# The k'v product of the batch two on follows the mean squares; four pairs of banks; the rest tokens go ahead of the fourth row tile

## The reference, cut to what matters

```
kv  = einsum('bhsd,bhse->bhde', k, v)              # 8 heads of 64; no softmax
out = einsum('bhsd,bhde->bhse', q, kv)
x   = out / sqrt(mean(out*out, -1) + 1e-6) * g_norm       # then heads side by side: [8, 576, 512]
u, v = split(relu(x @ w_in), 2, axis=-1)                  # 512 columns each
v_n  = (v - mean(v)) / sqrt(var(v) + 1e-6)
v_s  = einsum('ts,bsd->btd', w_spatial, v_n) + b_spatial[:, None]
y    = (u * v_s) @ w_out
h    = relu(y @ w_in2)                                    # w_out @ w_in2 is formed once
conv = three taps over the tokens of h
result = (h * sigmoid(conv)) @ w_out2
```

## Time and profile before

| | |
|---|---|
| median of 3 runs | 794.38 us (793.95 to 794.77) |
| the profiled execution's own time | 794.56 us |
| its span in the trace | 792.5 us |
| PE busy / ACT busy / DVE busy | 781.0 / 421.9 / 584.9 us |
| granted TensorE clock | full speed |
| one body of the steady loop | 47.0 us |

### The profile page before, as it was taken

How to read it: one execution, slowest core, us unless ns; L and a number is a source line. 1 busy time by engine, 2 the same in 40 slices (tenths; PEclk the granted TensorE clock), 3 DMA queues, 4 the chain that set the end, 5 groups by cost and what they waited for, 6 DMA issues and landing times.

```text
span 792.5 us, 15400 instructions
## 1 busy us (share of the span) xinstructions
PE 781.0 (99%) x5654; PEld 702.0 (89%) x5654; DVE 584.9 (74%) x1262; ACT 421.9 (53%) x753; POOL 29.5 (4%) x40
## 2 busy tenths in 40 slices
PE   8999999999999999999999999999999999999997
PEld 7679889798988979899899898898989999898986
DVE  3666776776577475666889989497995979679791
ACT  3664462544335254352556767366674756557562
POOL 4342000000000000000000000000000000000000
PEclk9999999999999999999999999999999999999999
DMA  9872455856334272222091213222022212102101
GB/s 316 308 256 61 150 199 193 301 181 224 105 103 181 74 268 60 104 51 80 36 355 67 105 54 105 67 75 84 1 105 67 104 53 86 71 13 105 53 0 66
DMA packets 35001, 96.86 MB, mean 122 GB/s; under 512 B 2738, under 2 KB 9106, under 8 KB 30228
## 3 DMA queue, kind: packets, MB, share of 16 engines
q1 hardware_dynamic: 33476, 90.09, 33.2%
q10 hardware_dynamic: 1488, 6.30, 2.1%
HBM read 66.11 MB, written 30.28 MB: 122 GB/s over the span
## 4 chain that ended last, share of the span: by engine, by line
PE 89%; DVE 6%; DMA 1%; ACT 1%; issue 1%; SPq 0%; DVEq 0%; ACTq 0%
PE ps L619 25%; PE ps L443 24%; PE ps L611 21%; PE ps L474 11%; PE ps L396 3%; PE ps L412 2%; PE ps L544 1%; DMA kv_raw<-kv_rest_dram 1%; PE ps L422 1%; DVE t_then_s L1148 1%; DVE bn_stats L1067 1%; DVE work L1087 1%; DVE v_hg_split L1093 1%; DVE vrr L1080 0%; PE ps L532 0%
## 5 line engine op out<-in xcount | busy, mean ns | idle before, releaser
L619 PE MATMUL ps<-w_in_split,v_hg_split 128*128 128x512 f32 x832 | 194.9, 390 | 0.0
L619 PEld LDWEIGHTS ps<-w_in_split,v_hg_split 128*128 128x128 f32 x832 | 155.7, 188 | 32.2
L443 PE MATMUL ps<-w_sp_split,v_hg_split 128*128 128x288 f32 x896 | 120.5, 295 | 1.0 <-DVE v_hg_split L1095 0.6
L443 PEld LDWEIGHTS ps<-w_sp_split,v_hg_split 128*128 128x128 f32 x896 | 119.3, 188 | 1.5 <-issue 0.8
L443 PE MATMUL ps<-x_operand_split,w_in_split 128*128 128x288 f32 x768 | 104.3, 296 | 1.6 <-ACT work L701 1.6
L443 PEld LDWEIGHTS ps<-x_operand_split,w_in_split 128*128 128x128 f32 x768 | 102.1, 188 | 3.7 <-ACT work L701 2.0
L474 PE MATMUL ps<-w_in_split,x_operand_split 128*128 128x512 f32 x384 | 93.6, 397 | 0.0
L474 PEld LDWEIGHTS ps<-w_in_split,x_operand_split 128*128 128x128 f32 x384 | 70.4, 188 | 20.9 <-issue 6.1
L1244 DVE TENSOR_TENSOR h_and_sums<-h_and_sums,ps 128x288 f32<-128x288 f32 x160 | 68.5, 450 | 7.5 <-PE ps L611 7.2
L1100 DVE TENSOR_TENSOR work<-ps,work 128x576 f32<-128x576 f32 x32 | 24.1, 757 | 59.4 <-PE ps L443 59.1
L1244 DVE TENSOR_TENSOR h_and_sums<-work,ps 128x288 f32<-128x288 f32 x64 | 28.2, 450 | 46.8 <-PE ps L611 46.3
(11 more groups left out here) (123 smaller groups left out, 1035.9 us busy)
## 6 DMA issues: line engine op xcount, KB each, us to landing
kv_raw<-kv_main_dram SPq DMA_DIRECT2D x8, 2048.0 KB, 10.2
q_raw<-q_T_dram SPq DMA_DIRECT2D x8, 1152.0 KB, 7.2
operand_scratch<-t_then_s SPq DMA_DIRECT2D x8, 1152.0 KB, 5.3
operand_raw<-operand_scratch SPq DMA_DIRECT2D x8, 1152.0 KB, 5.5
sq_then_r<-r_scratch SPq DMA_DIRECT2D x14, 576.0 KB, 6.2
operand_scratch<-work SPq DMA_DIRECT2D x24, 288.0 KB, 2.6
operand_more_raw<-operand_scratch SPq DMA_DIRECT2D x8, 864.0 KB, 7.2
w_out_split_scratch<-v_hg_split ACTq DMA_DIRECT2D x2, 2048.0 KB, 9.0
```

Source lines behind the costliest of these rows:

```text
L443: last = pe.matmul(pair[bank][:, c, :], st, mo[:, c * HALF:(c + 1) * HALF], start=(n == 0), stop=(n == len(steps) - 1))
L619: last = pe.matmul(PS[:, ROW_BANK[i], :], x, wout2[:, w, F_ORDER[e], :], start=(e == 0 and n == 0), stop=(e == FT - 1 and n == len(PASSES) ...
```

## The change

- The order on PE in a body is now: v tiles 0, 1, 2, the rest tokens, tile 3 (`V_TILES`), the squares, then `kv_product(b + 2)`, then the u products. `kv_product(1)` stands ahead of body 0. Bodies 0 to 5 hold a k'v product, bodies 6 and 7 none.
- `kv_copy(b + 2)` on ACT and DVE follows their work on the v tiles.
- A fourth pair of banks (6 and 7) is used for the first u product and the first spatial product, and the other pairs are dealt out anew. The rest tokens use bank 0, tile 3 bank 3.
- The waits follow from that: u product 1 waits for the relu of the rest tokens, u product 2 for that of tile 3, u product 3 for the mean squares and for both copies of k'v. Spatial product 1 waits for all four `u_relu`, spatial products 2 and 3 for nothing of their own.
- Body 6 stands outside the loop. The SP queue's code is not touched.

```diff
-U_PAIR = [0, 1, 2, 0]
-GATE_PAIR = [1, 2, 0, 1]
+U_PAIR = [3, 0, 1, 2]
+GATE_PAIR = [3, 2, 0, 1]
...
-V_BANK = [0, 1, 2, 3, 2]
+V_TILES = [0, 1, 2, FULL, 3]
+V_BANK = [0, 1, 2, 3, 0]
...
-        pair = [PS[:, 2 * i:2 * i + 2, 0:HALF] for i in range(3)]
+        pair = [PS[:, 2 * i:2 * i + 2, 0:HALF] for i in range(4)]
...
             def u_product(b, m, ahead):
-                if m == 0:
-                    pe.wait_ge(s_vr, b * NT + 2)
-                elif m == 1:
+                if m == 1:
+                    pe.wait_ge(s_vr, b * NT + 4)
+                elif m == 2:
                     pe.wait_ge(s_vr, (b + 1) * NT)
-                elif m == 2:
-                    if ahead:
-                        pe.wait_ge(s_ms, b + 2)
-                else:
-                    pe.wait_ge(s_ur, b * MT + 1)
+                elif m == 3 and ahead:
+                    pe.wait_ge(s_ms, b + 2)
...
             def spatial_product(b, m):
                 if m == 0:
                     pe.wait_ge(s_vlo, (b + 1) * NT)
-                if m < 3:
-                    pe.wait_ge(s_ur, b * MT + 2 + m)
-                else:
-                    pe.wait_ge(s_g, b * MT + 1)
+                    pe.wait_ge(s_ur, b * MT + 1)
+                if m == 1:
+                    pe.wait_ge(s_ur, b * MT + 4)
...
-            def body(b, ahead):
+            def body(b, ahead, two_ahead):
                 first = isinstance(b, int) and b == 0
-                if ahead:
-                    if first:
-                        pe.wait_ge(s_xm, MT)
-                    else:
-                        pe.wait_ge(s_g, b * MT - 2)
-                    kv_product(b + 1)
-                for i in range(NT):
+                for i in V_TILES:
+                    if i == FULL:
+                        v_rest_product(b)
+                        continue
                     v_product(b, i, ahead)
                     if ahead and i in (0, 2):
                         o_product(b + 1, i)
                         o_product(b + 1, i + 1)
                 if ahead:
                     square_sum(b + 1)
+                if two_ahead:
+                    kv_product(b + 2)
                 if first:
                     pe.wait_ge(s_winu, MT)
                 for m in range(MT):
+                    if m == 3 and two_ahead:
+                        pe.wait_ge(s_kvd0, b + 3)
+                        pe.wait_ge(s_kvd1, b + 3)
                     u_product(b, m, ahead)
...
-            body(0, True)
-            with pe.Fori(1, B - 1) as b:
-                body(b, True)
-            body(B - 1, False)
+            pe.wait_ge(s_xm, MT)
+            kv_product(1)
+            body(0, True, True)
+            with pe.Fori(1, B - 2) as b:
+                body(b, True, True)
+            body(B - 2, True, False)
+            body(B - 1, False, False)
```

More of the change, by code:

```diff
@@ L466, in v_product @@
[L466 to L469, removed]
-                        if i == 2:
[L471 to L474, removed]
+                steps = [(m, a, w) for m in range(MT) for a, w in PASSES]
@@ new lines, in v_product @@
+                for n, (m, a, w) in enumerate(steps):
+                    if n == len(steps) - 1:
+                        if i == 2:
+                            pe.wait_ge(s_xr, b + 1)
+                            pe.wait_ge(s_vr, b * NT + 1)
+                        if ahead:
+                            if i == 0:
+                                o_ready(b + 1, 1)
+                            if i == 2:
+                                o_ready(b + 1, 3)
+                            if i == 3:
+                                square_ready(b + 1)
+                    last = pe.matmul(PS[:, V_BANK[i], 0:F1], XG[:, a, m, i * P:(i + 1) * P], WA[:, w, m, F1:2 * F1],
+                                     start=(n == 0), stop=(n == len(steps) - 1))
@@ L475, in v_product, with v_rest_product @@
+                last.then_inc(s_v, 1)
+            def v_rest_product(b):
+                steps = [(m, w) for m in range(MT) for w in (HI, LO)]
+                for n, (m, w) in enumerate(steps):
+                    last = pe.matmul(PS[:, V_BANK[FULL], 0:F1], x_rest[:, m, :], WA[:, w, m, F1:2 * F1],
+                                     start=(n == 0), stop=(n == len(steps) - 1))
                 last.then_inc(s_v, 1)
             def u_product(b, m, ahead):
-                if m == 0:
-                    pe.wait_ge(s_vr, b * NT + 2)
-                elif m == 1:
+                if m == 1:
+                    pe.wait_ge(s_vr, b * NT + 4)
+                elif m == 2:
@@ L738, in body @@
                         sp_hi(i - 2)
-                    if ahead and i == FULL:
+                    if ahead and i == NT - 1:
                         root(b + 1)
@@ L869, in _ @@
             W_copy(7)
-            body(0, True)
-            body(1, True)
-            body(2, True)
-            with act.Fori(3, B - 1) as b:
-                body(b, True)
+            kv_copy(1)
+            body(0, True, True)
+            body(1, True, True)
+            body(2, True, True)
+            with act.Fori(3, B - 2) as b:
+                body(b, True, True)
+            body(B - 2, True, False)
             def operand_hi(b, k):
@@ L1229, in _ @@
             x_lo(0, 3)
-            body(0, True)
-            body(1, True)
-            body(2, True)
-            with dve.Fori(3, B - 1) as b:
-                body(b, True)
-            body(B - 1, False)
+            kv_copy(1)
+            body(0, True, True)
+            body(1, True, True)
+            body(2, True, True)
+            with dve.Fori(3, B - 2) as b:
+                body(b, True, True)
+            body(B - 2, True, False)
+            body(B - 1, False, False)
             def h_block(f, half):
```

94 lines of the change are left out of this document (44 added, 50 removed).

## The result

The changed kernel takes 803.54 us (median of 5, 803.03 to 805.07) against 794.69 for the kernel before in the same series: a ratio of 1.0115, 95% interval 1.0104 to 1.0125. It is 8.9 us slower, where I had forecast 3.1, and lies above the top of my range, 802.0. The direction was right and the size was not. One of my rivals had named about 804, with waits of 11.7 us for the loads; that its time fits is chance, since the waits for the loads were 4.0 us.

What follows compares the result with a forecast made beforehand. PE was taken as the bound, busy 781.0 of 792.5 us. Loads +4.8, switches -1.3, body 0 -1.3 and body 7 +0.9 made +3.1 us: 797.5 us against a median of 794.38, range 792.8 to 802.0.

Steps and rivals of the forecast that it cites:

- One of my rivals: Loads in the loop: queues take turns, q piles up, every body lands 2 us later; about 804 us, chance 0.11.
- the edits that cost nothing: Tile 0's x operand, first u product's banks, u products 1 to 3, fourth `u_relu`, DVE's statistics: no time lost.
- one wait stays: Body 0, bound from above: DVE and ACT get 0.8 us of copies in between, leaving a gain of only 0.6 us.
- Body 0: PE's waits of 0.67 us ahead of u product 1 and 0.65 ahead of the spatial products both go: -1.3 us.
- Body 7: Spatial product 1 waits for the fourth `u_relu`, 1.4 us later, less an earlier last split of v: +0.9 us (0 to +1.5).
- my discount of 0.5 for the single `v_hi`: Body 7: the last tile needs one `v_hi` instead of two, so the last split of v comes some 0.5 us earlier.
- buys nothing: Body 7: PE reaches spatial product 1 about 0.9 us sooner, as u product 1 no longer waits, with no gain.
- The loads: Bodies 1 to 5: PE waits for `kv_rest`, 3.5 us by present landings plus 1.3 for q's and ACT's loads: +4.8 us.
- a deadline of 16.5: Steady bodies: PE wants both loads of k and v 16.5 us after the end of the spatial products.
- The switches: Six bodies each lose one 0.22 us price of coming from small products to full-size matmuls: -1.3 us.

Runs made afterwards that it cites:

- e1: Changed kernel with DVE's copy of the k'v product of batch 2 taken in body 0 ahead of the mean squares; 798.74 us.
- e6: Kernel before with one wait added: u product 3 of body 0 waits for the last split of v; 799.55 us.
- e4: Changed kernel with the three edits of e1, e2 and e3 together; 790.18 us, ratio 0.9936 to the kernel before.
- e10: The same kernel as e4, measured again in another series; 790.45 us, ratio 0.9942 to the kernel before.
- e5: Changed kernel with the k'v product and its copies back at the start of a body, keeping the new banks and v tile order; 797.48 us.
- e2: Changed kernel with ACT's third and fourth `u_relu` of body 7 moved ahead of the weight splits; 798.95 us.
- e7: Changed kernel with the load of q issued only when the k'v product of the same body is through; 804.12 us.
- e8: Changed kernel with ACT's two loads of w_out2 (bodies 1 and 2) issued behind the last v tile, not the first; 802.47 us.
- e3: Changed kernel with the loads of k and v issued one body earlier, right behind the load of q in SP's list; 800.41 us.

## Why the prediction was wrong

**The step that failed is the one on the edits that cost nothing**: "u products 1 to 3 wait for relus, mean squares and copies that are due 2.4 us later than before." The copy of k'v was not due at all in that place before, and on DVE it stands behind the last split of v. In body 0 that split ended at 72.92 before (the chain of the kernel before), and the spatial products started right behind it:

```profile
72.22 0.70 DVE v_hg_split L1095
```

That is 31.0 us from the start of tile 0. The copies take 0.8 more by my own figure. By the earlier trace rows the v stage with a k'v product takes 19.24 us and three u products 72 x 0.133 = 9.6, so u product 3 is due at 28.8. That makes about 3.0 us of waiting, from rows of before alone. I used this very row to price a gain of 1.3 us, and allowed for the copies with at most 0.7 of it ("one wait stays"), but did not ask which u product now waits for them. Measured: a wait of 3.23 us, shown by e1.

**The clock was in no term.** Idle stretches on PE had been short before (0.67, 0.65, 0.39 us, and 0.88 in body 7), and the granted clock was full there, so that no row of before showed what a longer one costs. That was no reason to put a longer one at its own length. Behind waits of 3.2 and 2.7 us in the changed kernel, and of 3.7 us in e6, the clock was at half speed: 2.6 us more in body 0, 1.5 in body 7. Over all traces, the 14 waits of 2.4 to 3.7 us from body 0 on were each followed by half clock, and none of the waits of up to 1.7 us there was. The Trainium skill, page "TensorE: Matmul & The Clock Gate", section "Part 1: The HAM clock gate (the "warmup" mystery)", says that the gate is set by how busy the array has been recently and that an idle array goes back to 1.2 GHz. The traces agree with that. In e4 and e10, without such a wait, the clock stays full from body 0 until PE's work is done.

**Body 0**, forecast -1.3: +4.2 in the trace, from +3.2, +2.6 and the two old waits that did go. They went for one of the reasons that I gave, the 2.4 us of k'v product that stand ahead of both. The other reason, the rest tokens' earlier place, does not hold by itself: in e5, without a k'v product there, the late wait grew instead. In e4 the body takes 89.36 - 42.36 = 47.0 us with the moved product, 1.8 less than 46.31 + 2.48, which is the gain that I had forecast and 0.5 more.

**Body 7**, forecast +0.9: the mechanism and its own size were right, and the clock is what was missing. Spatial product 1 started 410.04 - 378.18 = 31.9 us into the body, against 401.01 - 370.35 = 30.7 before: +1.2, within my 0 to +1.5. Of my discount of 0.5 for the single `v_hi` only 0.2 came. The last split of v ended 21.5 us into the body and 21.6 before, since the rest tokens' two splits now stand ahead of the root for tile 3. The other 1.5 us of the 2.7 was clock. I had noted that PE arrives sooner than before and that this "buys nothing"; it made the wait 2.7 us long where 0.4 had been. Whether a shorter wait would have kept the clock up in this body was not tried.

**The loads**, forecast +4.8 with a deadline of 16.5: the deadline and nearly the sum were right, the split over the bodies was not. Deadline 256.80 - 240.25 = 16.55. The bodies from 1 to 6 are 2.9 longer with 0.2 saved in each, so the waits are about 4.1; PE's timeline has 1.2, 1.7 and 1.1 us in bodies 1, 2 and 3, where I had 2.1, 0.4 and 1.0. Landings, from issue: 11.9, 12.4, 11.8 and 10.0 us in bodies 1 to 4, against 12.8, 11.1, 11.7 and 9.8. The load in body 1 came 0.9 us sooner and that in body 2 1.3 later, so that the near agreement of the sum is luck in part; in e2 and e7 body 1 waits 2.4 and 2.5 us and pays for the clock as well, for which I had no term either. e8 puts bodies 1 and 2 on ACT's load, e7 a part of body 3 on q's. The Trainium skill's rule on turns between queues (page "DMA: Bandwidth & Descriptors", section "Queues, rings and completion order") agrees with e8: move the other queue's load away and `kv_rest` lands about 2 us earlier in bodies 1 and 2. That the queues take turns packet by packet no run here shows.

**The switches**, forecast -1.3: right, six times 0.2 us. Tile 0 takes 2.76 us and not 2.95, and the steady body 46.80 and not 47.0; the squares, the k'v product and the u products follow each other in 1.12, 2.48 and 27.76 us, as long as each had been.
**The sum by measured terms**: +4.1 loads, -1.2 switches, +4.2 in body 0 and +2.7 in body 7 make +9.8 for the profiled execution; with the 0.8 ahead of body 0 that is 10.6, and 10.5 is the difference. The median, 8.9, is lower. The other four executions had a granted clock of 0.996 and not 0.994, about 1.6 us less time lost to the clock, which is the difference between the two prices seen in body 0.

**What stays open**: why body 3's load lands later than those of bodies 4 and 5 in every trace that has the loads in their old place (11.0 to 11.8 us against 9.8 to 11.2), beside q's share; and why the fall of the clock takes 1.7 us of full-speed time in one execution and 3.4 in another, behind the same wait of 3.2 us.

## What to carry to other kernels

A product that is moved takes its consumers along: for every copy out of its bank, look up what stands ahead of it on its own engine in the body where that engine is latest, not only in the steady one. When a step moves to an earlier place, the load that feeds it must be moved in its queue as well; here the move earned 0.6% only once the load, one copy and two relus had followed it, and 0.1 of that comes from the relus alone. And do not price a stall on PE at its own length: here waits of 2.7 to 3.7 us cost 4.2 to 6.2 us, because the clock went with them.

## What the runs showed of the hardware

- Behind idle stretches of 2.4 to 3.7 us PE's granted clock was 0.50. The price was 1.7 or 3.4 us of full-speed time, also for one and the same wait of 3.2 us: 3.4 in the changed kernel, e2 and e8, 1.7 in e3 and e7.
- A k'v product of 40 small matmuls behind other small matmuls costs its 2.48 us and nothing more (bodies of 46.8 us); the same product between two groups of full-size matmuls costs 0.2 us more (bodies of 47.0 us).
- With a load of 1024 KB from ACT's queue issued at the same time, the end of 2304 KB from SP's queue came 11.7 to 13.1 us after the issue in body 1 and 12.2 to 12.4 in body 2 (four executions); with that load issued later it came after 9.8 and 10.2 (e8).
